# Moving the token sums, splitting two gate multiplications and moving one weight remainder in a fused attention and two-layer feed-forward kernel

## The chip, the cores and the metric

One Trainium2 chip, one core. The metric is the device time of one launch in microseconds (us); lower is better. Everything from the inputs in HBM to the output in HBM is one program.

## The reference

```python
# attention, 2 batches x 8 heads, 768 tokens, head size 64; hash buckets of 6 bits mask the scores
scores = np.where(mask, scale * q @ k.T, -1e9); attn = softmax(scores); x = attn @ v     # -> (1536, 512)
# layer 1: d_ff 1536
x = (1 / (1 + np.exp(-(x @ w_gate))) * (x @ w_val)) @ w_out
# layer 2: d_ff 2048, h = x @ w_in
g = np.where(h >= 1, h, np.where(h <= -1, 0.0, (h + 1) ** 2 / 4))
out = g @ w_out2
```

All of it is fp32. The kernel splits each operand of a large matrix product into a high part and a rest (both in TensorE's fp32 format) and adds three products.

## The kernel before, in words

There are three stages on one core. The first is attention: 96 steps (`STEPS`), 12 for each of eight pairs of heads (pair `i`, step `u` of the pair). In a step TensorE computes one block of scores, turns the probabilities of five steps before, and weighs values; VectorE empties scores, ScalarE takes the exponential, GpSimd (POOL in the profile) normalises (L491) and, in gaps, prepares the next stage: `first_set` splits the first weights (L540, L541), `first_sum` forms token sums (L567 to L575).

The two feed-forward layers run in 40 *sets*. Sets 0 to 23 belong to layer 1, even ones to the gate and odd ones to the value; sets 24 to 39 belong to layer 2. `FIRSTS = (0, 12, 24, 32)` begin the four *groups* (a layer and a batch of 768 tokens). A set widens the tokens to 256 hidden columns. It is a 2x2 block product done with seven products instead of eight (`product(n, r)`, r = 0 to 6; L748 to L750, six matmuls each). For that the token blocks and the weight blocks are first added and subtracted: the *token sums* are `sum_x(g, k)` on VectorE, four for each group to come, and the weight sums are `sums_a` and `sums_b` on GpSimd. GpSimd then makes the rests of the rounded weights: `low_a`, `low_s` (L522), and for the output weights `low_wo` (L529).

Products go to two PSUM banks in turn, so that product r waits until product r-2 has been emptied. ScalarE empties product 0 (`first_product`, L986), VectorE the others (`empty`, L1275 and L1282; for r = 4 two instructions). Between products TensorE does units of the narrowing product (`down`; L777, L778 in layer 1, L788 to L790 in layer 2), in a fixed order (`units`); they wait for the tile's rest (`rest_tile`, L1286) and for `wo_split`.

A gate set ends with two sigmoids on ScalarE. A value set multiplies them in: `gate_quarter` (L1295), `gate_second` (L1301, 768 columns), `gate_first` (L1306, 384 columns). A set of layer 2 has for each of its two tiles a `clamp` (L1313, VectorE), a relu (L996) and a square (L999, both ScalarE, together `hinge_part`), and an addition (`add_hinge`, L1317, VectorE). `empty(n, 1)` also needs the set's `first_product` and, after a value set, its last gate multiplication.

Each engine runs its own list in order, and semaphores join them. ScalarE's `hinge_set(n)` for layer 2 is, in order: `first_product(n)`, `round_tile`, `hinge_part`, `round_tile`, `round_w(n + 1)` (L952, L953, L955), then in odd sets `round_wo2(n)` (L960), then `hinge_part` of the set's first tile. The output weights come two tiles at a time into one part of a staging tile, `stage[:, 2]`, of which there is one only: ScalarE rounds it (`round_wo`, waits for `wo_in`), GpSimd takes the rest (`low_wo`, adds to `wo_split`), and then the queue on SP loads the next (L403), in this order for set n:

```python
sp.wait_ge(w_split, 2 * (n - 1))
load_w(n)
...
if WO2 < n <= WO2 + T2 and n % 2 == 0:      # WO2 = 15, T2 = 16
    f = (n - WO2 - 1) // 2
    sp.wait_ge(wo_split, T1 // 2 + f)       # T1 = 12
    load_wo(wo2_v, f)
```

Of the kernel before, what the change touches and what calls it, by code (L numbers as in the profile page):

```python
# [12 lines left out]
ALU = mybir.AluOpType  # L13
# [9 lines left out]
def build(nc, q, k, v, proj, w_gate, w_val, w_out, w_in, w_out2, out):  # L23
# [39 lines left out]
    with ctx:  # L63
# [132 lines left out]
        def group_of(n):  # L196
            return sum(n >= first for first in FIRSTS) - 1
# [262 lines left out]
        def _(pool):  # L460
# [101 lines left out]
            def first_sum(k, half=None):  # L562

                b11, b12, b21, b22 = (block_x(0, a, c) for a, c in ((0, 0), (0, 1), (1, 0), (1, 1)))
                dst = early[:, k]
                if k == 0:
                    pool.tensor_tensor(dst, b22, b12, ALU.subtract).then_inc(x0_sums, 1)  # L567
                if k == 1:
                    pool.wait_ge(x0_sums, 3)
                    pool.tensor_tensor(dst, early[:, 0], b11, ALU.add).then_inc(x0_sums, 1)  # L570
                if k == 2:
                    pool.tensor_tensor(dst[:, half], b12[:, half], b11[:, half], ALU.subtract).then_inc(x0_sums, 1)
                if k == 3:
                    pool.wait_ge(x0_sums, 4)
                    pool.tensor_tensor(dst[:, half], b21[:, half], early[:, 1, half], ALU.subtract).then_inc(x0_sums, 1)  # L575
# [38 lines left out]
            for g in range(STEPS + HT):  # L614
                i, u = g // U, g % U
                if g % HT == 0 and g:
                    sums(g // HT - 1)
                if g >= HT:
                    normalise(g - HT)
                if g % HT == 0 and 12 <= g < STEPS:  # L620
                    add_half((g - 12) // HT, g - HT + 1)
                if g < STEPS and g % T == 2:
                    split_v(g // T)
                if u == late(i) + 5 and i < NP - 1:
                    scale_codes(i + 1)
                if 1 <= i < 7 and u == 11:

                    first_set(i - 1)
                if i == NP - 3 and u in (4, 7, 10):
                    first_sum(0 if u == 4 else 2, (u - 7) // 3)  # L630
                if i == NP - 2 and u in (4, 7, 10):
                    first_sum(1 if u == 4 else 3, (u - 7) // 3)
                if i == NP - 1 and u % 3 == 1:
                    first_high(HIGH0_POOL[u // 3])
# [6 lines left out]
            for n in range(2, NSETS):  # L641
                if n - 1 in FIRSTS[1:]:

                    pool.wait_ge(x_low, R * (group_of(n) + 1))
                sums_a(n)
                sums_b(n)
                low_a(n)
                low_s(n)
                if n % 2 == 0 and n <= N1 // 2:
                    f = n // 2 - 1  # L650
                    low_wo(f, f, (narrow(2 * f + 1), narrow(2 * f)))
                if WO2 + 1 < n <= WO2 + T2 + 1 and n % 2:
                    f = (n - WO2 - 2) // 2
                    low_wo(T1 // 2 + f, f, (narrow2(2 * f), narrow2(2 * f + 1)))

# [232 lines left out]
        def _(act):  # L888
# [91 lines left out]
            def first_product(n):  # L980
                act.wait_ge(p_done, R * n + 1)
                if n:
                    act.wait_ge(*emptied(n - 1, 2))
                    if widens(n - 1) == "value":
                        act.wait_ge(half_gated, pair_of(n - 1) + 1)
                act.copy(u1[:, :], bank(n, 0)).then_inc(e_act, 1)  # L986
# [4 lines left out]
                    act.wait_ge(*emptied(n, 6 - second))  # L991
                    act.activation(hidden(pp, second), hidden(pp, second), ACT.Sigmoid).then_inc(sig_done, 1)

            def hinge_relu(t):
                act.wait_ge(clamped, t - TILES1 + 1)
                act.activation(tile(t), tile(t), ACT.Relu, bias=minus_one).then_inc(hinge_parts, 1)  # L996

            def hinge_square(t):
                act.activation(tmp[:, :], tmp[:, :], ACT.Square, bias=half, scale=0.5).then_inc(hinge_parts, 1)  # L999

            def hinge_part(t):
                hinge_relu(t)
                hinge_square(t)

            def empty_y(g):

# [45 lines left out]
            def hinge_set(n):  # L1052
                t, g = 2 * pair_of(n), group_of(n)
                ahead = n + 1 in FIRSTS
                if n - 1 not in FIRSTS:
                    first_product(n)
                if n in FIRSTS:
                    round_w(n + 1)
                    empty_y(g - 1)

                    hinge_relu(t)
                    first_product(n + 1)
                    hinge_square(t)
                    return
                round_tile(t - 2)
                hinge_part(t - 1)
                if ahead:
                    round_x(g + 1, 0)
                    round_x(g + 1, 1)
                round_tile(t - 1)  # L1070
                if n + 1 < NSETS:
                    round_w(n + 1)
                if n < WO2 + T2 and n % 2 and not ahead:
                    round_wo2(n)
                if ahead:
                    for r in (2, 3, 4):
                        round_x(g + 1, r)
                hinge_part(t)
                if ahead:
                    round_tile(t)  # L1080
                    hinge_part(t + 1)
                    round_x(g + 1, 6)
                    round_tile(t + 1)
                    round_x(g + 1, 5)
# [60 lines left out]
        def _(dve):  # L1145
# [151 lines left out]
            def gate_second(n):  # L1297
# [2 lines left out]
                dve.wait_ge(*emptied(n, 5))  # L1300
                dve.tensor_tensor(two, two, tmp[:, :], ALU.mult).then_inc(gated, 1)  # L1301

            def gate_first(n):
                one = hidden(pair_of(n), 0)
                dve.wait_ge(*emptied(n, 6))
                dve.tensor_tensor(one[:, G:S], one[:, G:S], u2, ALU.mult).then_inc(gated, 1)  # L1306
# [11 lines left out]

            def sum_ahead(n):

                g = group_of(n)
                if g < 3 and n - FIRSTS[g] in (3, 4, 5):
                    sum_x(g + 1, n - FIRSTS[g] - 3)

            def gate_set(n):
                t, g = 2 * pair_of(n), group_of(n)
# [12 lines left out]
            def value_set(n):  # L1339
                t, g = 2 * pair_of(n), group_of(n) + 1  # L1340
                empty(n, 1)
                empty(n, 2)
                gate_quarter(n)
                empty(n, 3)
                empty(n, 4)
                sum_ahead(n)
                empty(n, 5)
                if n - 1 in FIRSTS or n + 1 in FIRSTS:

                    gate_second(n)  # L1350
                    empty(n, 6)
                else:
                    empty(n, 6)
                    gate_second(n)
                gate_first(n)
                if n + 1 in FIRSTS:
                    rest_tile(t)
                    rest_x(g, 0)
                    rest_tile(t + 1)
                    rest_x(g, 1)  # L1360
                    sum_x(g, 3)
                    for r in MADE[2:]:
                        rest_x(g, r)

            def hinge_set(n):
                t, g = 2 * pair_of(n), group_of(n)
                ahead = n + 1 in FIRSTS
                if n - 1 not in FIRSTS:
                    empty(n, 1)
                if n - 1 in FIRSTS:  # L1370

                    empty(n, 2)
                    rest_tile(t - 2)
                    empty(n, 3)
                    add_hinge(t - 1)
                else:
                    if n not in FIRSTS:
                        rest_tile(t - 2)
                        add_hinge(t - 1)
                    empty(n, 2)  # L1380
                    empty(n, 3)
                    if n not in FIRSTS:
                        rest_tile(t - 1)
                if ahead:
                    rest_x(g + 1, 0)
                empty(n, 4)
                if n - 1 in FIRSTS:
                    rest_tile(t - 1)
                sum_ahead(n)
                empty(n, 5)  # L1390
                clamp(t)
                if ahead:
                    rest_x(g + 1, 1)
                empty(n, 6)
                if n in FIRSTS:
                    empty(n + 1, 1)
                add_hinge(t)
                clamp(t + 1)
                if ahead:
                    rest_tile(t)  # L1400
                    sum_x(g + 1, 3)
                    add_hinge(t + 1)
                    rest_x(g + 1, 2)
                    rest_tile(t + 1)
                    for r in MADE[3:]:
                        rest_x(g + 1, r)
# [82 lines left out]
```

## Time and profile before

| | us |
|---|---|
| median of 3 runs | 792.86 (792.75 to 793.1) |
| the profiled execution | 792.82 |
| its span | 790.7 |
| TensorE (PE) busy | 775.2, 98% |
| VectorE (DVE) busy | 551.3, 70% |
| ScalarE (ACT) busy | 461.5, 58% |
| GpSimd (POOL) busy | 538.5, 68% |

Products of the sets start at about 243 us of the span; group 1 starts at 392, group 2 at 534 and group 3 at 661. A row of a timeline gives the start and the length in us, the engine, the line, the operation and its tiles; in brackets stands the idle time of the engine before it, and what ended it. An instruction that waits for something after it has been started is counted as busy.

### The profile page before, as it was taken

Reading aid. Unit: us, or ns where it says so; the run is one execution under the profiler, and the core shown is the slowest. Engines: PE = TensorE matmul, PEld = TensorE weight load, DVE = VectorE, ACT = ScalarE, POOL = GpSimd, SP = SyncE. Lnnn points to the kernel's source line nnn. Section 1 sums busy time; section 2 is a strip of 40 time slices with the busy share of each in tenths; the row PEclk is TensorE's granted clock in tenths of the full one; section 3 lists DMA queues with packets and bytes.
Section 4 is the critical chain, followed back from the end, with each engine's and each line's share of the span. In section 5 each row is a group of like instructions: output and inputs, shape, how many; then the busy total and the mean of one; then the engine's idle time right before and its main releaser. Section 6 shows DMA issues by size and latency. Waiting matters only on the chain.

```text
span 790.7 us, 12182 instructions
## 1 busy us (share of the span) xinstructions
PE 775.2 (98%) x4403; PEld 717.3 (91%) x4403; DVE 551.3 (70%) x862; ACT 461.5 (58%) x731; POOL 538.5 (68%) x533
## 2 busy tenths in 40 slices
PE   7999999999999999999999999999999999999998
PEld 6899999998989999999899999988899988899996
DVE  5888888888888666555765655577677776766554
ACT  4888988988997443344453334356455465634443
POOL 4567667778889988877596977747756755465420
PEclk9999999999999999999999999999999999999999
DMA  6895586385100222022021211121121011201002
GB/s 146 181 197 131 136 168 141 79 163 131 55 1 1 80 81 81 29 78 80 27 81 54 80 54 63 44 80 54 32 77 54 29 51 40 95 27 54 1 1 80
DMA packets 61930, 60.08 MB, mean 76 GB/s; under 512 B 28384, under 2 KB 51632, under 8 KB 61872
## 3 DMA queue, kind: packets, MB, share of 16 engines
q1 hardware_dynamic: 61712, 59.32, 28.5%
q8 instruction: 35, 0.57, 0.3%
q14 instruction: 23, 0.19, 0.1%
q10 hardware_dynamic: 160, 0.00, 0.0%
HBM read 37.75 MB, written 3.15 MB: 52 GB/s over the span
## 4 chain that ended last, share of the span: by engine, by line
PE 79%; DVE 6%; ACT 6%; issue 4%; POOL 4%; DMA 0%; SPq 0%; DVEq 0%; POOLq 0%; ACTq 0%
PE ps L748 12%; PE ps L749 11%; PE ps L750 11%; PE ps L777 8%; PE ps L789 5%; PE ps L790 5%; PE ps L788 5%; PE ps L778 4%; PE ps L714 4%; ACT ph L906 2%; PE ps L731 2%; PE ps L732 2%; PE ps L702 2%; DVE probs L1207 2%; PE ps L705 2%
## 5 line engine op out<-in xcount | busy, mean ns | idle before, releaser
L748 PE MATMUL ps<-xop,wset 128*128 128x384 f32 x560 | 191.0, 341 | 4.1 <-DVE u L1282 2.1
L749 PE MATMUL ps<-xop,wset 128*128 128x384 f32 x560 | 189.3, 338 | 0.0
L750 PE MATMUL ps<-xop,wset 128*128 128x384 f32 x560 | 188.8, 337 | 0.0
L1282 DVE TENSOR_TENSOR u<-ps,u 128x384 f32<-128x384 f32 x144 | 79.6, 553 | 109.0 <-PE ps L750 108.3
L516 POOL TENSOR_TENSOR wset<-stage,wset 128x512 fp32r<-128x512 f32 x39 | 56.5, 1448 | 112.7 <-ACT wset L953 112.7
L748 PEld LDWEIGHTS ps<-xop,wset 128*128 128x128 f32 x560 | 105.2, 188 | 18.0 <-issue 3.8
L1218 DVE TENSOR_TENSOR pl<-ps,ph 128x768 fp32r<-128x768 f32 x96 | 91.5, 954 | 26.5 <-ACT ph L906 25.4
L749 PEld LDWEIGHTS ps<-xop,wset 128*128 128x128 f32 x560 | 105.4, 188 | 3.5
L491 POOL TENSOR_SCALAR probs<-probs,small 128x768 f32<-128x768 f32 x96 | 88.4, 927 | 24.9 <-DVE small L1212 22.1
L750 PEld LDWEIGHTS ps<-xop,wset 128*128 128x128 f32 x560 | 105.2, 188 | 0.0
L522 POOL TENSOR_TENSOR wset<-wsum,wset 128x1024 fp32r<-128x1024 f32 x39 | 95.3, 2443 | 0.0
L1207 DVE TENSOR_SCALAR_CACHE_REDUCE probs<-ps 128x768 f32<-128x768 f32 x96 | 90.9, 949 | 5.2 <-PE ps L705 4.6
L910 ACT ACTIVATE probs<-probs,small 128x768 f32<-128x768 f32 x96 | 90.0, 937 | 7.7 <-DVE probs L1207 7.4
L906 ACT CAST ph<-ps 128x768 fp32r<-128x768 f32 x96 | 76.7, 800 | 21.4 <-PE ps L714 19.9
L714 PE MATMUL ps<-ident,probs 128*128 128x128 f32 x576 | 78.9, 273 | 2.1 <-DVE probs L1207 1.2
L1282 DVE TENSOR_TENSOR hid<-ps,u 128x384 f32<-128x384 f32 x84 | 46.6, 555 | 46.8 <-PE ps L750 45.2
L790 PE MATMUL ps<-wo,hl 128*128 128x512 f32 x192 | 75.3, 392 | 0.0
L714 PEld LDWEIGHTS ps<-ident,probs 128*128 128x128 f32 x576 | 67.2, 140 | 9.0 <-issue 3.8
L789 PE MATMUL ps<-wo,hh 128*128 128x512 f32 x192 | 75.3, 392 | 0.0
L777 PE MATMUL ps<-hh,wo 128*128 128x512 f32 x192 | 75.2, 397 | 0.0
L788 PE MATMUL ps<-wo,hh 128*128 128x512 f32 x192 | 74.9, 390 | 0.0
L986 ACT COPY u<-ps 128x384 f32<-128x384 f32 x40 | 19.1, 478 | 93.7 <-PE ps L750 93.7
(134 smaller groups left out, 1710.4 us busy)
## 6 DMA issues: line engine op xcount, KB each, us to landing
stage<-in_moe_w_in_dram SPq DMA_DIRECT2D x16, 512.0 KB, 3.6
stage<-in_moe_w_out_dram SPq DMA_DIRECT2D x14, 512.0 KB, 3.6
stage<-in_moe_w_gate_dram SPq DMA_DIRECT2D x12, 512.0 KB, 4.3
stage<-in_moe_w_val_dram SPq DMA_DIRECT2D x12, 512.0 KB, 3.5
ops<-qh SPq DMA_DIRECT2D x15, 384.0 KB, 5.3
ops<-kh SPq DMA_DIRECT2D x28, 192.0 KB, 5.1
qn<-in_q_dram SPq DMA_DIRECT2D x16, 192.0 KB, 4.5
kn<-in_k_dram SPq DMA_DIRECT2D x16, 192.0 KB, 5.0
```

The costliest lines, as they stand in the source:

```text
L522: pool.tensor_tensor(weights(n, 1)[:, 3:7], wsum[:, :], weights(n, 0)[:, 3:7].bitcast(F32), ALU.subtract).then_inc(w_split, 1)
L714: last = pe.transpose(dst[:, t * P:(t + 1) * P], probs[n % RING][:, t * P:(t + 1) * P], ident[:, :])
L748: pe.matmul(dst, high[:, c, :], high_x(r)[:, c, :], start=(c == 0), stop=False)
L749: pe.matmul(dst, high[:, c, :], low_x(r)[:, c, :], start=False, stop=False)
L750: last = pe.matmul(dst, low[:, c, :], high_x(r)[:, c, :], start=False, stop=(c == 1))
L777: pe.matmul(main, w[:, cols], h[:, t % 3, 0:512], start=(first and n == 0), stop=(last_tile and n == 2))
L788: pe.matmul(ps[:, r, :], hh[:, t % 3, rows], wh, start=first, stop=False)
L789: pe.matmul(ps[:, r, :], hh[:, t % 3, rows], wl, start=False, stop=False)
L790: last = pe.matmul(ps[:, r, :], hl[:, t % 3, rows], wh, start=False, stop=last_tile)
L906: act.copy(dst, turned_slot("T", n).rearrange("p (t n) -> p t n", t=T)).then_inc(pt_high, 1)
L1207: dve.tensor_scalar(probs[g % RING].rearrange("p (s n) -> p s n", s=2), score_slot(g), NO_MATCH, None, ALU.min, ALU.min, accum_out=lowest( ...
L1282: dve.tensor_tensor(dst, bank(n, r), other, ALU.add).then_inc(e_dve, 1)
```

## The change

- `first_sum` in the sixth pair of heads (`i == NP - 3`) runs in steps 1, 4 and 7 instead of 4, 7 and 10.
- In groups 0 and 1 the token sums 0, 1, 2 for the next group move from the sets 3, 4, 5 of a group to its sets 4, 6, 8, all of them gate sets. Value sets form none. Group 2 keeps 3, 4, 5.
- In a group's second and last value set (sets 1, 11, 13, 23) the gate multiplication of 768 columns becomes two of 384: one before `empty(n, 5)`, one after.
- In the first set of groups 2 and 3 (24, 32) relu and square follow each other on ScalarE, and the next set's `first_product` comes after them; on VectorE `add_hinge` comes ahead of the next set's `empty(n + 1, 1)`.
- On GpSimd the `low_wo` that followed the weights of set 25 (`N1 + 1`) follows those of set 26.

```diff
-                if i == NP - 3 and u in (4, 7, 10):
-                    first_sum(0 if u == 4 else 2, (u - 7) // 3)
+                if i == NP - 3 and u in (1, 4, 7):
+                    first_sum(0 if u == 4 else 2, u // 7)
...
-                if WO2 + 1 < n <= WO2 + T2 + 1 and n % 2:
+                if WO2 + 1 < n <= WO2 + T2 + 1 and (n % 2 and n != N1 + 1 or n == N1 + 2):
...
             def hinge_set(n):
-                if n - 1 not in FIRSTS:
-                    first_product(n)
+                first_product(n)
                 if n in FIRSTS:
                     round_w(n + 1)
                     empty_y(g - 1)
-                    hinge_relu(t)
-                    first_product(n + 1)
-                    hinge_square(t)
+                    hinge_part(t)
                     return
...
+            def gate_half(n):
+                two = hidden(pair_of(n), 1)
+                dve.wait_ge(sig_done, 2 * pair_of(n) + 1)
+                dve.wait_ge(*emptied(n, 4))
+                dve.tensor_tensor(two[:, G:S], two[:, G:S], tmp[:, G:S], ALU.mult)
+
+            def gate_other(n):
+                two = hidden(pair_of(n), 1)
+                dve.wait_ge(*emptied(n, 5))
+                dve.tensor_tensor(two[:, 0:G], two[:, 0:G], tmp[:, 0:G], ALU.mult).then_inc(gated, 1)
...
-                if g < 3 and n - FIRSTS[g] in (3, 4, 5):
-                    sum_x(g + 1, n - FIRSTS[g] - 3)
+                at = (4, 6, 8) if g < 2 else (3, 4, 5) if g == 2 else ()
+                if n - FIRSTS[g] in at:
+                    sum_x(g + 1, at.index(n - FIRSTS[g]))
...
                 empty(n, 4)
-                sum_ahead(n)
-                empty(n, 5)
                 if n - 1 in FIRSTS or n + 1 in FIRSTS:
-                    gate_second(n)
+                    gate_half(n)
+                    empty(n, 5)
+                    gate_other(n)
                     empty(n, 6)
                 else:
+                    empty(n, 5)
                     empty(n, 6)
                     gate_second(n)
...
                 empty(n, 6)
+                add_hinge(t)
                 if n in FIRSTS:
                     empty(n + 1, 1)
-                add_hinge(t)
                 clamp(t + 1)
```

## Rows read from the trace of the kernel before

**Rows 1.** The page, part 1: busy time, share of the span, instructions

```profile
PE 775.2 (98%) x4403; PEld 717.3 (91%) x4403; DVE 551.3 (70%) x862; ACT 461.5 (58%) x731; POOL 538.5 (68%) x533
```

**Rows 2.** Waits of PE, whole span: us in total, times, longest

```profile
PE ps L748 <- DVE u L1282: 2.1, 9, 0.4
PE ps L748 <- DVE hid L1282: 1.8, 3, 0.9
```

**Rows 3.** Timeline, 180 to 190 us, GpSimd and TensorE, attention

```profile
180.54 1.02 POOL L572 TENSOR_TENSOR early<-x 128x384 f32<-128x384 f32 x1
...
184.83 0.90 POOL L491 TENSOR_SCALAR probs<-probs,small 128x768 f32<-128x768 f32 x1 [0.30 <-DVE small L1212]
...
185.73 0.84 PE L714 MATMUL ps<-ident,probs 128*128 128x128 f32 x6 [0.76 <-POOL probs L491]
```

**Rows 4.** Timeline, 262 to 267 us, end of set 1: GpSimd, VectorE, TensorE

```profile
262.36 2.39 POOL L522 TENSOR_TENSOR wset<-wsum,wset 128x1024 fp32r<-128x1024 f32 x1
264.71 3.56 POOL L529 TENSOR_TENSOR wo<-stage,wo 128x512 fp32r<-128x512 f32 x2
...
264.27 1.29 DVE L1301 TENSOR_TENSOR hid<-hid,tmp 128x768 f32<-128x768 f32 x1
...
264.43 0.33 PE L750 MATMUL ps<-xop,wset 128*128 128x384 f32 x1
264.60 0.34 PE L748 MATMUL ps<-xop,wset 128*128 128x384 f32 x1
...
266.18 0.41 PE L748 MATMUL ps<-xop,wset 128*128 128x384 f32 x1 [0.37 <-DVE u L1282]
```

**Rows 5.** Timeline, 404 to 410 us, end of set 13: GpSimd, VectorE

```profile
405.04 2.39 POOL L522 TENSOR_TENSOR wset<-wsum,wset 128x1024 fp32r<-128x1024 f32 x1
...
407.00 1.24 DVE L1301 TENSOR_TENSOR hid<-hid,tmp 128x768 f32<-128x768 f32 x1
```

**Rows 6.** Timeline, sets 3 to 4 and 17 to 18

```profile
286.85 1.15 DVE L1239 TENSOR_TENSOR xt<-x 128x768 f32<-128x768 f32 x1
...
290.72 1.09 DVE L1306 TENSOR_TENSOR hid<-hid,u 128x384 f32<-128x384 f32 x1
...
292.56 0.44 PE L748 MATMUL ps<-xop,wset 128*128 128x384 f32 x1 [0.37 <-DVE u L1282]
...
455.15 0.41 PE L748 MATMUL ps<-xop,wset 128*128 128x384 f32 x1
```

**Rows 7.** Timeline, sets 24 and 25, and the same product of set 33

```profile
540.61 2.84 POOL L529 TENSOR_TENSOR wo<-stage,wo 128x512 fp32r<-128x512 f32 x2
...
540.76 1.55 DVE L1313 TENSOR_SCALAR tmp<-hid 128x768 f32<-128x768 f32 x1
...
547.22 0.44 PE L748 MATMUL ps<-xop,wset 128*128 128x384 f32 x1 [0.91 <-DVE hid L1282]
...
673.85 0.44 PE L748 MATMUL ps<-xop,wset 128*128 128x384 f32 x1 [0.56 <-DVE hid L1282]
```

**Rows 8.** Timeline, sets 25 and 26, and the page's DMA issues

```profile
551.09 1.05 ACT L955 CAST wset<-wsum 128x1024 fp32r<-128x1024 f32 x1
552.05 1.13 ACT L960 CAST wo<-stage 128x512 fp32r<-128x512 f32 x2
...
553.92 0.92 ACT L999 ACTIVATE tmp<-tmp,small 128x768 f32<-128x768 f32 x1
...
553.54 2.40 POOL L522 TENSOR_TENSOR wset<-wsum,wset 128x1024 fp32r<-128x1024 f32 x1
...
543.48 0.37 SPq L403 DMA_DIRECT2D stage<-in_moe_w_out_dram  x1
...
560.82 0.34 PE L748 MATMUL ps<-xop,wset 128*128 128x384 f32 x1
...
stage<-in_moe_w_out_dram SPq DMA_DIRECT2D x14, 512.0 KB, 3.6
```

**Rows 9.** Timeline, TensorE's first instructions

```profile
1.52 3.25 PE L830 MATMUL ps<-ident 128*128 128x128 f32 x14 [1.52 <-POOL ident L463]
```

More of the change, by code:

```diff
@@ L992, in sigmoids, with hinge_part @@
                     act.activation(hidden(pp, second), hidden(pp, second), ACT.Sigmoid).then_inc(sig_done, 1)
-            def hinge_relu(t):
+            def hinge_part(t):
                 act.wait_ge(clamped, t - TILES1 + 1)
                 act.activation(tile(t), tile(t), ACT.Relu, bias=minus_one).then_inc(hinge_parts, 1)
-            def hinge_square(t):
                 act.activation(tmp[:, :], tmp[:, :], ACT.Square, bias=half, scale=0.5).then_inc(hinge_parts, 1)
-            def hinge_part(t):
-                hinge_relu(t)
-                hinge_square(t)
             def empty_y(g):
@@ L1059, in hinge_set @@
                     empty_y(g - 1)
-                    hinge_relu(t)
-                    first_product(n + 1)
-                    hinge_square(t)
+                    hinge_part(t)
                     return
```

## The prediction

> **What bounds the kernel now.** I read the page's busy times first: TensorE is busy 98% of the span [rows 1], so time can leave only where it waits, or come where it is made to wait. The waits of TensorE give these places: nine waits for VectorE's emptying into `u`, 2.1 us in all, three for emptying into `hid`, 1.8 us [rows 2], and one of 0.76 us for GpSimd in attention [rows 3]. The timeline then names the product behind each. The bracket understates a wait: matmuls of a product start 0.17 apart (264.43, 264.60), so products follow each other every 1.05 us, while 264.60 and 266.18 are 1.58 apart with only 0.37 in the bracket [rows 4]; the true loss there is 0.53. I count losses from start to start. The sum is made against the profiled execution, 792.82 us with a span of 790.7; the median, 792.86, is the same within 0.1. A measurement can't tell less than 0.2% (1.6 us) from no change.
>
> **1. `first_sum` moved (attention).** The half sum at step 10 takes 1.02 us on GpSimd at 180.54, ahead of the weights' split and of the normalising that starts at 184.83; TensorE gets its probabilities at 185.73, after 0.76 idle [rows 3]. In step 7 nothing waits for the other half today, and in step 1 GpSimd has idle time behind it. Taken out, the normalising ends about 1.0 earlier, which is more than the idle: I take -1.0 (bounds -0.76 and -1.06; zero if step 1 has no room).
>
> **2. Gates by halves in set 1.** The row at 264.27 is the key. GpSimd's `low_s` runs 262.36 to 264.75; `gate_second` is started at 264.27 but ends at 265.56, 0.81 after `low_s`; `low_wo`, queued at 264.71, is held in turn [rows 4]. So a VectorE instruction with both inputs in SBUF and a GpSimd one exclude each other for a whole instruction; emptying, with one input in PSUM, doesn't take part. `gate_half` is queued after the fourth emptying, about 263.5, in the middle of `low_s`: it ends at 264.75 plus half of 0.81, 265.16. Behind it in VectorE's list is `empty(1, 5)`, which until now came first: it ends at about 265.65, so product (2,0) starts at 265.75 instead of 264.60 [rows 4]. Then GpSimd's waiting `low_wo` goes first (about 1.15 more, 266.3), `gate_other` ends at 266.7, `empty(1, 6)` at 267.2, product (2,1) starts at 267.3 instead of 266.18. Sum +1.1. If the halves met no lock it would be -0.4, the shorter work ahead of `empty(1, 6)`; with one more GpSimd instruction between, +1.5.
>
> The Trainium skill ("SBUF — State Buffer", section "SBUF: two separate sides") says that the port pair shared by VectorE and GpSimd is locked by whoever starts first for its full instruction, against the idea that both slow down in proportion. The trace agrees: 0.81 after `low_s`'s end. By sharing in proportion `gate_half` would end near 264.6 and this term would be +0.5 instead.
>
> **3. The same in sets 13, 11 and 23.** Set 13: `low_s` runs 405.04 to 407.43, `gate_second` ends at 408.24 [rows 5] and `empty(13, 6)` follows. Now `gate_half` (queued at about 406.5) ends at 407.84, `empty(13, 5)` at 408.3, the next GpSimd instruction, a `sums_a`, gets the port for 0.6, `gate_other` ends at 408.85, and so `empty(13, 6)` starts 0.6 later than now: +0.6 (bounds -0.2, +0.9). Sets 11 and 23 are followed by 12 units of `down`, some 12.9 us in which TensorE needs only the rests of two tiles; the gates shift by -0.1 and +0.7, the cover is 0.3 for the first tile and 4 for the second: 0.
>
> **4. Token sums out of the value sets.** In set 3 the sum (286.85, 1.15 us) holds the port and pushes GpSimd's weight sums back by 0.7, so that the last of them meets `gate_first` at 290.72 (1.09 instead of about 0.55); `empty(4, 1)` is late and product (4,3) starts after 0.37 idle [rows 6]. Without it `gate_first` ends at about 291.4 instead of 291.81: -0.4. Set 5 is alike: -0.4. In set 17 the sum stands ahead of `empty(17, 5)`, and product (18,0) starts at 455.15 [rows 6], 0.3 late: -0.3. In the gate sets 6, 8, 18, 20 a sum of up to 2.9 us (with the lock) stands ahead of `empty(n, 5)`, but there units of `down` lie between products and leave over 1 us; set 4 carries one today without a wait. Sum -1.1 (bounds -1.4, -0.2).
>
> **5. Relu and square in a row.** In set 24 `clamp` is locked out by `low_wo` (540.76, 1.55 long), which the change moves away, and relu, `first_product`, square and `add_hinge` follow late; product (25,4) starts at 547.22 [rows 7]. New: `clamp` ends 541.3, square 543.1, `first_product(25)` 543.5, `add_hinge(24)` 544.1, `clamp(25)` 545.1, `empty(25, 2)` 545.6, product (25,4) 545.7. That is 1.5 us early, and ScalarE's `round_w(26)` comes 1.5 early too. In set 33 the same product starts at 673.85 [rows 7] and comes at about 673.3: -0.6 (bounds -0.8, 0). The later `first_product` costs at most 0.1.
>
> **6. `low_wo` moved from 25 to 26: the decisive step.** The staging part for output weights is single. The load that SP issues in set 26 waits for `wo_split` 11, and the eleventh `low_wo` is the one moved. Today SP issues it at 543.48 [rows 8], at the end of the pair that begins at 540.61 [rows 7], and ScalarE rounds it at 552.05 [rows 8] without waiting. Now this `low_wo` is behind `low_s(26)`, which needs ScalarE's `round_w(26)` of the same set; and right behind `round_w(26)` ScalarE wants the load. So it waits out the whole loop. With the 1.5 of step 5: `round_w(26)` ends at 552.14 - 1.55 = 550.6; `low_s(26)` at 555.94 - 1.55 = 554.4; two `low_wo` without a lock, 2.5, to 556.9; SP issues at once; landing after 3.6 [rows 8], 560.5. ScalarE stands for 9.9 us. Queued behind are the rounding (1.0), relu, square (to 2.8 after 552.05 today [rows 8]) and `first_product(26)`: square ends 563.3, `first_product` 563.7. Product (26,2) waits for that: 563.8, against 560.82 [rows 8] less 1.55 = 559.3. TensorE stands 4.5 us; ScalarE's slack before this product is 5.4 us today: square ends at 554.84 [rows 8], `first_product` would end 0.5 later, and the product starts at 560.82.
>
> It isn't over then. The unit of `down` after (26,2) needs `rest_tile(26)`, behind `add_hinge(26)`, `clamp(27)` and `empty(26, 1)` on VectorE, while the weights of set 27, loaded behind the late load on SP's queue, land at about 561.9 and GpSimd's sums take the port in turns: 567.0 or so instead of 565. And `empty(26, 2)` waits behind `add_hinge(27)`. I get product (26,4) at 569.6, today 564.3: +5.3 net of step 5's gain in set 25. Bounds: 4.3 (no lock, TensorE catches up at 568.6) and 6.6 (the load takes 4.2, each VectorE instruction is locked out). The next load has its old order, and nothing more is late.
>
> **Sum:** -1.0 + 1.1 + 0.6 + 0 - 1.1 - 0.6 + 5.3 = +4.3; 792.8 + 4.3 = 797.1 us.
>
> **Rivals.** *A, the lock spares the halves* (`low_s` ends before they are queued, as everything shifts): steps 2 and 3 become -0.6 in place of +1.7, 794.8 us. For it: the phase of GpSimd against VectorE decides; against: `low_s` and the fourth emptying both follow TensorE's products, and so keep their phase.
>
> *B, TensorE's clock falls in the stall.* At the kernel's start 14 transposes take 3.25 us [rows 9], 0.21 apart; in attention six take 0.84 [rows 3], 0.11 apart: the first is the 1.2 GHz level. After 4.5 us of standing still the clock may be at that level again, and half of the slow time is lost; the slow stretch at the start lasts at least the 3.25 us, with the next transposes some 5.8, which gives 1.6 to 2.9, so about 799.3 us. Against it: no idle time now in the feed-forward stage is over 0.91, so no row speaks. The Trainium skill ("TensorE: Matmul & The Clock Gate", section "HAM oscillation — how this bites in real kernels") says that an idle wait in a kernel's middle throttles it again; no row before shows that, and it gets the chance below.
>
> *C, the late load reaches nobody: faster.* If ScalarE's wait is under its slack of 5.4 us (a load that lands by 556), the stall at (26,2) is gone and step 5's -1.5 in set 25 stays: 792.8 - 1.0 + 1.1 + 0.6 - 1.1 - 0.6 - 1.5 = 790.3. For it: today this very load lands before ScalarE wants it (543.48 + 3.6 against 552.05 [rows 8]). Against: the order of SP, GpSimd and ScalarE above leaves 9.9, nearly twice the slack.
>
> *D, the gate sets' sums hurt:* each of four could be late by up to 0.5 if the lock takes longer than 2.9: +1, 798.
>
> **How the numbers follow.** Forecast 0.58, A 0.12, B 0.16, C 0.07, D 0.07. The range 794.6 to 799.8 holds A, D and most of B. Slower by over 0.2%: all but C and a little of A with every gain at its bound: 0.91; same 0.03; faster 0.06.
>
> **What would show it.** Step 1: no wait of L714 for L491. Step 2: L748 waits for DVE near 264 and 266, with L1282 late behind a locked 384-column multiplication. Step 4: no waits at products (4,3), (6,3), (18,0). Step 5: no wait at (25,4), (33,4). Step 6: ACT L960 waits some 10 us for DMA `stage<-in_moe_w_out_dram`, issued at about 555 to 557, and PE L748 waits over 4 us for ACT `u` L986. If ACT waits under 5 us there, the prediction is wrong in its largest term. The clock column shows B.

## The result, and the profile after

The changed kernel takes 799.34 us (median of 6 runs, 798.26 to 801.74) against 792.59 for the kernel before, a ratio of 1.0087 (95% interval 1.0072 to 1.0101): slower by 0.9%. The profiled execution took 798.61 us, its span 796.8. The forecast was 797.1 with a range of 794.6 to 799.8.

TensorE's waits of the changed kernel, whole span (us in all, times, longest). TensorE's and ScalarE's lines are shifted by one, VectorE's by more: L749 to L751 are the products, L987 is `first_product`, L1273 `empty`, L1277 `rest_tile`.

```profile
PE ps L749 <- ACT u L987: 4.4, 1, 4.4
PE ps L749 <- DVE tmp L1273: 1.7, 2, 1.0
...
PE ps L789 <- DVE hl L1277: 1.3, 1, 1.3
...
PE ps L749 <- DVE u L1273: 1.1, 5, 0.3
```

The three waits for `hid` of [rows 2] are gone, and the nine for `u` are five. In their place stand three new kinds: one of 4.4 us for ScalarE, one of 1.3 for a tile's rest, two for `tmp`, which is what the product after the halved gates waits for. Here is where the 4.4 comes from, on ScalarE, GpSimd and SP (compare [rows 8]; L961 is `round_wo`, L504 the first of the weight sums for set 27):

```profile
548.25 1.05 ACT L956 CAST wset<-wsum 128x1024 fp32r<-128x1024 f32 x1
559.28 1.14 ACT L961 CAST wo<-stage 128x512 fp32r<-128x512 f32 x2 [9.98 <-DMA stage<-in_moe_w_out_dram]
...
561.99 0.45 ACT L987 COPY u<-ps 128x384 f32<-128x384 f32 x1
...
560.74 0.73 POOL L504 TENSOR_TENSOR wsum<-stage 128x256 f32<-128x256 f32 x1 [5.15 <-DMA stage<-in_moe_w_in_dram]
...
555.62 0.37 SPq L403 DMA_DIRECT2D stage<-in_moe_w_out_dram  x1
```

ScalarE's `round_w(26)` ends at 549.3 and it stands for 10 us. What it stands for is told by the chain of waits of the changed kernel, in order of time (start, us, what):

```profile
548.42 1.30 POOL wset L516
549.72 1.01 POOL wset L518
550.73 2.36 POOL wset L522
...
554.30 1.30 POOL wo L529
555.62 3.58 DMA stage<-in_moe_w_out_dram
...
559.80 0.61 ACT wo L961
...
561.25 0.83 ACT tmp L998
562.11 1.55 DVE hid L1320
...
565.13 0.88 DVE hl L1277
566.05 0.79 PE ps L789
```

The chain that sets the end isn't on TensorE from 540.3 to 566.05, 26 us; its second half, shown here, goes through GpSimd's rests, the load (3.58 us, as in [rows 8]), ScalarE and VectorE. TensorE, the same stretch:

```profile
562.49 0.69 PE L749 MATMUL ps<-xop,wset 128*128 128x384 f32 x1 [4.36 <-ACT u L987]
562.98 0.52 PE L750 MATMUL ps<-xop,wset 128*128 128x384 f32 x1
563.30 0.52 PE L751 MATMUL ps<-xop,wset 128*128 128x384 f32 x1
...
566.05 0.79 PE L789 MATMUL ps<-wo,hh 128*128 128x512 f32 x1 [1.27 <-DVE hl L1277]
...
569.09 0.39 PE L751 MATMUL ps<-xop,wset 128*128 128x384 f32 x1
...
570.00 0.34 PE L749 MATMUL ps<-xop,wset 128*128 128x384 f32 x1
```

After the stall the matmuls start 0.32 apart (562.98, 563.30) instead of 0.17, until 569.1. The windows view of the changed kernel has it in the column PEclk, the seventh (busy times of PE, PEld, DVE, ACT, POOL ahead of it):

```profile
556.00:562.40 6.40, 2.14 (x11) 1.56 (x9) 0.29 (x1) 3.12 (x5) 1.66 (x3) 1.00 0.73 246
562.40:569.20 6.80, 5.44 (x15) 4.65 (x16) 4.92 (x6) 4.35 (x8) 1.76 (x2) 0.50 0.01 2
...
```

So TensorE ran at 1.2 GHz for 6.8 us, having stood still for 4.4 us before. That is the forecast's rival B on top of its main line.

The end of set 1, which answers to [rows 4] (L1299 is `gate_half`, L1304 `gate_other`):

```profile
260.70 2.39 POOL L522 TENSOR_TENSOR wset<-wsum,wset 128x1024 fp32r<-128x1024 f32 x1
263.05 3.14 POOL L529 TENSOR_TENSOR wo<-stage,wo 128x512 fp32r<-128x512 f32 x2
...
261.84 1.67 DVE L1299 TENSOR_TENSOR hid<-hid,tmp 128x384 f32<-128x384 f32 x1
263.43 0.54 DVE L1273 TENSOR_TENSOR tmp<-ps,u 128x384 f32<-128x384 f32 x1
264.00 1.05 DVE L1304 TENSOR_TENSOR hid<-hid,tmp 128x384 f32<-128x384 f32 x1
...
264.12 0.41 PE L749 MATMUL ps<-xop,wset 128*128 128x384 f32 x1 [0.99 <-DVE tmp L1273]
...
265.67 0.41 PE L749 MATMUL ps<-xop,wset 128*128 128x384 f32 x1 [0.27 <-DVE u L1273]
```

`gate_half`, half of a multiplication, takes 1.67 us, longer than the whole one of before (1.29): it is queued 1.1 us after `low_s` has started, where the whole one was queued 1.9 after, and it ends 0.42 after `low_s`.

The two traces can be laid against each other from product to product. I summed, set by set, by how much each matmul starts later than the usual distance after the one before it; the difference of after and before, in us:

| where | forecast | measured |
|---|---|---|
| attention, start of pair 7 to start of pair 8 | -1.0 | 30.17 before, 29.18 after: -0.99 |
| set 1 to 2 (halves) | +1.1 | +1.12 |
| set 13 to 14 (halves) | +0.6 | +0.65 |
| sets 4, 6, 18 (token sums) | -1.1 | -0.57 - 0.43 - 0.34 = -1.34 |
| sets 24, 25 (gone waits) | -1.5 | -1.54 |
| set 33 | -0.6 | -0.66 |
| set 26 (late load) | +6.8 | +8.53 |

The rows add up to +4.3 forecast and +5.8 measured. Set 26 alone is worth more than the whole loss. (The forecast's +5.3 was net of the 1.5 of set 25; the table has them apart.) The medians differ by 6.75, and the last 1.0 us of that is in no step. Outside the table, the first scores start 0.7 earlier in the profile of after and the last store lands 1.1 later; such differences come without any change: the kernel of run 4 below, the same up to there, starts its first product at 243.1, the changed one at 241.2.

### The profile page after: what moved, and what is told of

Its sections match the earlier page's. It is cut to its first block, busy times and chain, and to the rows that moved or that the text cites. A ratio compares the mean times of both kernels' runs of the same rounds, so it can differ in the third digit from the quotient of the medians.

```text
span 796.8 us, 12190 instructions
## 1 busy us (share of the span) xinstructions
PE 776.4 (97%) x4403; PEld 718.3 (90%) x4403; DVE 557.8 (70%) x866; ACT 461.1 (58%) x731; POOL 536.7 (67%) x533
## 4 chain that ended last, share of the span: by engine, by line
PE 78%; DVE 7%; ACT 6%; issue 4%; POOL 3%; DMA 1%; SPq 0%; DVEq 0%; POOLq 0%; ACTq 0%
PE ps L749 12%; PE ps L750 11%; PE ps L751 11%; PE ps L778 8%; PE ps L789 5%; PE ps L791 5%; PE ps L790 5%; PE ps L779 4%; PE ps L715 4%; ACT ph L907 3%; PE ps L732 2%; PE ps L733 2%; DVE probs L1198 2%; PE ps L703 2%; ACT probs L911 2%
## 5 line engine op out<-in xcount | busy, mean ns | idle before, releaser
L749 PE MATMUL ps<-xop,wset 128*128 128x384 f32 x560 | 191.6, 342 | 7.5 <-ACT u L987 4.4
L751 PE MATMUL ps<-xop,wset 128*128 128x384 f32 x560 | 189.3, 338 | 0.0
L1273 DVE TENSOR_TENSOR u<-ps,u 128x384 f32<-128x384 f32 x144 | 79.6, 553 | 103.1 <-PE ps L751 102.5
L749 PEld LDWEIGHTS ps<-xop,wset 128*128 128x128 f32 x560 | 105.6, 189 | 21.1 <-ACT u L987 5.1
L751 PEld LDWEIGHTS ps<-xop,wset 128*128 128x128 f32 x560 | 105.7, 189 | 0.0
L732 PE MATMUL ps<-ph,v 128*128 128x384 f32 x192 | 72.2, 376 | 0.1
L987 ACT COPY u<-ps 128x384 f32<-128x384 f32 x40 | 19.1, 477 | 91.2 <-PE ps L751 91.2
```

Of the source, the lines that this page charges most:

```text
L749: pe.matmul(dst, high[:, c, :], high_x(r)[:, c, :], start=(c == 0), stop=False)
L751: last = pe.matmul(dst, low[:, c, :], high_x(r)[:, c, :], start=False, stop=(c == 1))
```

## The experiments

My theory was that without the late load the kernel would not be slower, and that the load costs its time through ScalarE's list and then through the clock; that the halves cost because of the port that VectorE and GpSimd share; and that all the rest gains. The rivals stand with each run. Ratios are to the kernel before on the same chip, which took 792.74 us in the first four runs and 792.09 in the last four.

**1. The `low_wo` put back behind set 25, all else as changed.**

```diff
-                if WO2 + 1 < n <= WO2 + T2 + 1 and (n % 2 and n != N1 + 1 or n == N1 + 2):
+                if WO2 + 1 < n <= WO2 + T2 + 1 and n % 2:
```

> The changed kernel with its one moved output-weight remainder (low_wo) back behind the weights of set 25; all else as changed. Theory (ScalarE waits about 10 us for the late load, and that alone makes the kernel slower): the wait of L961 for the DMA is gone, product (26,2) doesn't wait, the clock stays at 2.4 GHz, and what is left is the sum of the other parts: -1.0 attention, +1.1 and +0.6 halves, -1.3 token sums, -0.7 set 33, -0.5 in set 25 (its clamp is locked out again): 790.8 us. Rival (the loss is spread over the halves and the reordering too): 794 or more.

791.96 us, ratio 0.9989 (0.9981 to 0.9998). The wait of ScalarE for a DMA, the stall and the low clock are gone; the kernel is now level with the one before or a little faster. The loss as a whole goes with this one edit; the costs and gains of the others come to about -0.9 us together. The forecast was 1.2 lower than the time. Half a us of that is set 25, which gained nothing; the rest isn't explained. VectorE's timeline of this kernel shows why (L1316 `clamp(24)`, L1320 `add_hinge(24)`, L1273 the emptying that product (25,3) waits for):

```profile
539.35 1.57 DVE L1316 TENSOR_SCALAR tmp<-hid 128x768 f32<-128x768 f32 x1
...
542.75 1.51 DVE L1320 TENSOR_TENSOR hid<-hid,tmp 128x768 f32<-128x768 f32 x1 [1.36 <-ACT tmp L998]
544.19 0.55 DVE L1273 TENSOR_TENSOR u<-ps,u 128x384 f32<-128x384 f32 x1
```

With the `low_wo` there, `clamp` is locked out as before (1.57), and the new order puts `add_hinge`, locked out as well (1.51), ahead of an emptying that the old order did first.

**2. The kernel before with only the `low_wo` moved.**

```diff
-                if WO2 + 1 < n <= WO2 + T2 + 1 and n % 2:
+                if WO2 + 1 < n <= WO2 + T2 + 1 and (n % 2 and n != N1 + 1 or n == N1 + 2):
```

> The kernel before with nothing but that low_wo moved from set 25 to set 26. Theory: ScalarE waits 10 us, TensorE 4.5 us at (26,2) and 1.5 us at the next unit of down, the clock is at the lower level for some 7 us (about 2.4 us lost); set 25 gains about 1.0, since its clamp is not locked out: 792.6 + 8.5 - 1.0 = 800.1 us. Rival (the stall needs the reordered relu and square as well): 795 or less.

800.86 us, ratio 1.0099 (1.0086 to 1.0112). Its ScalarE and TensorE waits:

```profile
ACT wo L960 <- DMA stage<-in_moe_w_out_dram: 10.2, 1, 10.2
...
PE ps L748 <- ACT u L986: 4.6, 1, 4.6
```

The stall needs nothing else of the change. Set 25 gained 0.89, the part of the -1.5 that comes from `clamp` being free; the reordering gives the other 0.65, but, by run 1, only when the `low_wo` isn't there. In this profile the clock stays at the lower level for 10.2 us (0.50 in the window 563.0 to 573.2), not 6.8, after a stall only 0.2 longer. The length of that stretch seems to differ from execution to execution, and the time with it: of this kernel's four, two have a mean granted clock of 0.996 and took 800.26 and 800.30 us, two have 0.993 (one is the profiled one) and took 801.41 and 801.45. In the changed kernel three with 0.994 took 798.26 to 799.03, three with 0.993 took 799.64 to 801.74. Only one of each has a profile, and what sets the length of the stretch was not tested.

**3. TensorE kept at work in the stall.**

```diff
+                    if (n, r) == (N1 + 2, 2):
+                        for _ in range(38):
+                            pe.matmul(ps[:, 1, 0:P], zero[:, :], zero[:, :], start=False, stop=False)
                     product(n, r)
```

> The changed kernel with 38 matmuls of a zero block added by TensorE ahead of product (26,2), into a sum that they leave as it is; at 0.11 us each (as the transposes in attention) they take 4.1 us, within the stall of 4.4. Theory (the stall lets TensorE's clock fall, which costs about 2.4 us on top of it): granted clock 1.0 throughout, matmuls of (26,2) and (26,3) 0.17 apart instead of 0.32, product (26,2) at the same time: 799.3 - 2.4 = 796.9 us. Rival (the slow matmuls are the remains of waits on weights or buffers): no change, 799.3 us, or more.

798.74 us, ratio 1.0069 (1.0057 to 1.0081) against 1.0087 for the changed kernel. TensorE's timeline of this kernel, with the added matmuls first, and its clock in the window of 562 to 569 us:

```profile
558.33 4.36 PE L879 MATMUL ps<-zero 128*128 128x128 f32 x38
562.98 0.44 PE L749 MATMUL ps<-xop,wset 128*128 128x384 f32 x1 [0.29 <-ACT u L990]
563.26 0.34 PE L750 MATMUL ps<-xop,wset 128*128 128x384 f32 x1
...
566.48 0.50 PE L789 MATMUL ps<-wo,hh 128*128 128x512 f32 x1 [2.17 <-DVE hl L1280]
...
569.00 0.34 PE L749 MATMUL ps<-xop,wset 128*128 128x384 f32 x1
```

```profile
562.00:569.00 7.00, 4.54 (x26) 3.83 (x24) 5.62 (x8) 4.61 (x7) 2.60 (x3) 1.00 0.00 1
```

In this profile the clock stays at 1.00, and the matmuls are 0.17 apart again. From product (26,2) to (26,4) it takes 6.0 us (562.98 to 569.00) instead of 7.5 (562.49 to 570.00), and set 26 as a whole, reckoned as in the table above, loses 7.2 instead of 8.5: the clock costs 1.3 to 1.5 us. I had said 2.4, adding up the slow matmuls. Part of them is hidden: the wait for the tile's rest grows from 1.3 to 2.2, for it ends when VectorE is through, however fast TensorE has come there. The price rests on these two traces and not on the times. The ratios are 0.0018 apart, 1.4 us, but their intervals overlap, and this kernel's executions are mixed: three have a mean clock of 0.999 or 1.0 (797.43, 797.69 and 799.28 us), two of 0.996 (798.74 and 798.96). So the clock fell somewhere in those two all the same; they have no profile, and where it fell is open.

**4. ScalarE takes the late load one set later.** GpSimd and SP as in the changed kernel.

```diff
-                if n < WO2 + T2 and n % 2 and not ahead:
+                if n < WO2 + T2 and n % 2 and not ahead and n != N1 + 1:
                     round_wo2(n)
+                if n == N1 + 2:
+                    round_wo2(n - 1)
```

> The changed kernel, but ScalarE takes the late load (the rounding of output weights 11) behind its round_w(27) in set 26 instead of behind round_w(26) in set 25. GpSimd's and SP's order are as changed, so the load is just as late. Theory (the time is lost because relu, square and first_product(26) queue behind the wait): no wait of ScalarE for the DMA, no stall at (26,2): 792.6 - 2.8 = 789.8 us. Rival (the late load or the late weights of set 27 behind it on SP's queue hurt by themselves): a stall of 1 us or more stays in sets 26 to 28, 791 or more.

790.73 us, ratio 0.9975 (0.9965 to 0.9984). With a load at least as late as in the changed kernel but without relu, square and `first_product(26)` queued behind it, a loss of 0.9% becomes a gain of 0.25%, 2.0 us. So it was what stands in ScalarE's list behind the wait that cost the time, and not the late load itself. The rival had a point as well, in the waits of this kernel:

```profile
ACT wset L953 <- DMA stage<-in_moe_w_in_dram: 3.9, 1, 3.9
...
PE ps L789 <- DVE hl L1279: 0.5, 1, 0.5
PE ps L749 <- POOL wset L518: 0.2, 1, 0.2
```

The weights of set 27 stand behind the late load on SP's queue; ScalarE waits 3.9 us for them, and 1.3 us of it come through to TensorE at the start of set 27 and in it. The forecast was 789.8, 0.9 lower than the time, in the direction of these 1.3 us. They may be fewer in most executions: the profiled one is the slowest of its kernel (793.42 us), and its late load took 4.46 us to land, in the changed kernel's profile 3.58. In the changed kernel it is GpSimd that waits for these weights, until 560.74 (above); what that adds to the longer wait was not taken apart.

**5. The kernel before with only the halves** (`gate_half` and `gate_other` around `empty(n, 5)`, as in the change).

> The kernel before with nothing but the gate multiplication of sets 1, 11, 13 and 23 in halves. Theory (GpSimd's low_s locks VectorE out of the port, and the emptying of product 5, which needs no port, is now queued behind the locked half): product (2,0) 1.1 us late, product (14,0) 0.8 late, 0.6 of it left, nothing in sets 11 and 23: 792.7 + 1.7 = 794.4 us. Rival (the halves free the last emptying sooner and only the changed kernel's other edits made them late): 792.3 or less.

794.71 us, ratio 1.0030 (1.0018 to 1.0041): a loss by itself, +2.4 (1.4 to 3.2). From product to product it is +1.1 at set 2 and +0.6 at set 14, 1.7 as forecast, and -0.1 in set 4 and -0.2 in set 11, which were not. The trace's sum is 1.4, at the lower end of the interval.

**6. The kernel before with only the token sums moved** (`first_sum` and `sum_ahead` as in the change).

> The kernel before with nothing but the token sums moved: first_sum to the steps 1, 4, 7 and the other sums to sets 4, 6, 8 of groups 0 and 1. Theory: -1.0 in attention, -0.55 before set 4, -0.45 before set 6, -0.35 before set 18: 792.7 - 2.3 = 790.4 us. Rival (the sums, locked out by low_s in the gate sets, are late for the next set): 791.5 or more.

789.88 us, ratio 0.9969 (0.9957 to 0.9981), -2.5. The gain is as large as worked out (-2.3), and no sum is late for anything in the gate sets.

**7. GpSimd made quiet beside the halves.** Run 1's kernel, leaving out the rests of the summed weights of sets 2 and 14 and of the first output weights: zeros are written instead.

```diff
+                if n in (2, 14):
+                    pool.memset(weights(n, 1)[:, 3:7].rearrange("p a c m -> p (a c m)").bitcast(mybir.dt.uint32), 0).then_inc(w_split, 1)
+                    return
...
+                    if k == 0:
+                        last = pool.memset(low.bitcast(mybir.dt.uint32), 0)
```

> The first experiment (changed kernel, low_wo back behind set 25), in which GpSimd writes zeros instead of the rests in low_s of sets 2 and 14 and in the first low_wo: instructions that read nothing from SBUF, and shorter. It leaves out these rests of the weights. Theory (lock): gate_half(1) and gate_half(13) run in 0.55 instead of up to 1.67, products (2,0) and (14,0) hardly wait: 792.0 - 1.3 = 790.7 us. Rival (two instructions and their waits in place of one make VectorE's list too long ahead of the fifth emptying, whatever GpSimd does): set 2 still 1 us late, 792.0 us.

789.76 us, ratio 0.9968 (0.9956 to 0.9980), against 0.9989 for run 1. GpSimd and VectorE of this kernel (L1305 `gate_half`, L1310 `gate_other`):

```profile
260.69 0.95 POOL L523 MEMSET wset<- 128x1024 uint32 x1
261.58 0.99 POOL L533 MEMSET wo<- 128x512 uint32 x2
262.54 0.73 POOL L504 TENSOR_TENSOR wsum<-stage 128x256 f32<-128x256 f32 x1
...
261.85 0.56 DVE L1305 TENSOR_TENSOR hid<-hid,tmp 128x384 f32<-128x384 f32 x1
...
262.91 0.78 DVE L1310 TENSOR_TENSOR hid<-hid,tmp 128x384 f32<-128x384 f32 x1
```

The same `gate_half`, queued at the same time (261.85; 261.84 in the changed kernel), takes 0.56 instead of 1.67, though GpSimd is at work in just that time (L533, two writes that read nothing), and the two writes aren't held up either: they take 0.99 for 1024 columns, the single one before them 0.95. That matters because the zeros are also quicker to write than `low_s` was to compute (0.95 against 2.39), so that L523 is over when `gate_half` starts; the evidence is L533 beside it. `gate_other` meets an addition that reads, and takes 0.78. Product (2,0) is no longer late (+0.04), and set 2 ends 0.2 earlier than in the kernel before; set 14 is level (+0.06). So it is the lock by an instruction of GpSimd that reads SBUF, not the number of VectorE's instructions.

**8. The gates whole again, the moved `low_wo` behind set 24.**

```diff
-                if WO2 + 1 < n <= WO2 + T2 + 1 and (n % 2 and n != N1 + 1 or n == N1 + 2):
-                    f = (n - WO2 - 2) // 2
+                if WO2 + 1 < n <= WO2 + T2 + 1 and (n % 2 and n != N1 + 1 or n == N1):
+                    f = (n - WO2 - 2) // 2 + (n == N1)
...
-                    gate_half(n)
                     empty(n, 5)
-                    gate_other(n)
+                    gate_second(n)
                     empty(n, 6)
```

> The changed kernel with the gate multiplications whole again, and with the moved low_wo put behind the weights of set 24 (an earlier place, in GpSimd's idle time before group 2) instead of set 26. Theory: the parts that gain stay, -1.0 attention, -1.3 sums, -1.5 set 25, -0.7 set 33, and both losses are gone: 792.7 - 4.5 = 788.2 us. Rival (the low_wo in the last sets of group 1 locks out rest_x on VectorE and makes the tokens of group 2 late): a new wait at the products of set 24, 789 or more.

788.46 us, ratio 0.9959 (0.9943 to 0.9975): the lowest median of all, -3.3 us (-2.0 to -4.5) where -4.5 was forecast. The 788.2 that I wrote was reckoned from 792.7, and this series' kernel before took 792.09, so the closeness of the two times is luck. The traces show 0.3 of what is missing: set 25 gained 1.21 instead of 1.5. Its whole list of TensorE's waits from the first product on is one line:

```profile
PE ps L749 <- DVE u L1273: 1.1, 5, 0.4
```

## Why the prediction was right

The direction and the place held, and the mechanism of nearly every step; the time was 2.2 us short of the median, and the loss 2.45 us too small (+4.3 forecast, +6.75 measured).

*Step 1* held to 0.01 us. *Step 2*: `gate_half` ends 0.42 after `low_s` (forecast half of 0.81), product (2,0) is 1.15 late and set 2 1.12, as worked out; run 7 shows that the lock is the cause, which before was read from one row. The step's wording was both too wide and too narrow: a memset of GpSimd doesn't take part (run 7), and `clamp`, with one input from SBUF, does. It took 1.55 us beside `low_wo` [rows 7] and 0.56 in the changed kernel (at 539.46, started just ahead of GpSimd's next instruction, which then took 1.14 instead of 0.73). Step 5 counted on that. The two rows, of VectorE and GpSimd of the changed kernel:

```profile
539.46 0.56 DVE L1316 TENSOR_SCALAR tmp<-hid 128x768 f32<-128x768 f32 x1
...
539.48 1.14 POOL L504 TENSOR_TENSOR wsum<-stage 128x256 f32<-128x256 f32 x1
```

*Step 3* held: +0.65 at set 14, nothing at 11 and 23. *Step 4* was 0.2 too small. *Step 5* held in the changed kernel, -1.54 and -0.66, but the share that I laid on the order of relu and square was not its own: in run 1 it gives nothing in set 25, in run 2 the freed `clamp` alone gives 0.89. *Rivals A, C and D* didn't come: the halves were locked, ScalarE's wait reached TensorE, and no gate set lost time to a sum.

*Step 6*: ScalarE's wait is 9.98 (forecast 9.9), TensorE's stall from start to start 4.51 (forecast 4.5). The term that was mis-sized is the rest of set 26: product (26,4) at +5.3 net was forecast; measured are +7.0 (570.00 against 564.3, with TensorE 1.3 early at the start of set 24). Run 3 splits the difference: with the clock kept up it is +5.6 (569.00, with TensorE 0.9 early), so 0.3 of the error is the sum itself. The other 1.4 is the lower clock, which the sum put at nothing and which I had as rival B with 0.16 and at 2.2 us. That B's total, 799.3, is the measured median is luck: its term was 0.8 too large, and 1.0 us of the difference between the medians is in no step. I had put it low because no row of the kernel before has TensorE idle for long. That was no evidence against it. The row that I did have, slow matmuls after nothing had run at the start [rows 9], pointed the way. The Trainium skill's rule ("TensorE: Matmul & The Clock Gate", section "HAM oscillation — how this bites in real kernels"), that an idle wait in mid-kernel throttles TensorE again, is what the clock column of the changed kernel shows: 0.50 after the 4.4 us.

## What to carry to other kernels

When an instruction is moved on one engine, follow the semaphore it raises through the other queues, load queues too, until it comes back to what the moved instruction itself waits for: a single buffer that is filled, rounded, used up and filled again had some 5 us of slack (landed at 547.0, wanted at 552.05 [rows 8]), and one place later in one list made it a chain that GpSimd, SP's queue, the transfer and ScalarE had to run through in turn, with relu, square and the next emptying standing behind it. Before splitting an instruction in two so as to start it sooner, look at what runs on the engine that shares its port at the new start time: the half took longer than the whole, and held up an emptying that needs no port. Price a forecast stall of TensorE with its clock: here 4.4 us of standing still cost 1.3 to 1.5 more.

## What was unexpected

The lower clock lasted 6.8 us in one profile and 10.2 in another, after stalls of 4.4 and 4.6 us; why is open. And a GpSimd memset does not lock VectorE out: a multiplication with both inputs in SBUF ran in 0.56 us beside two of them, where beside the subtraction of `low_s` it took 1.67. That agrees with the Trainium skill ("SBUF — State Buffer", section "SBUF: two separate sides"), which has VectorE's instructions with two SBUF inputs shut out only by GpSimd instructions that read SBUF.
